# A fused attention and routed-expert kernel: group table ahead of places, group 1's weights asked for sooner, group 0's output in two halves, later sources marked beside group 1

## The reference

```python
attn_out = _attn_ref(...)                                  # B=4, H=8, S=576, D=64, causal softmax + linear memory
x = attn_out.transpose(0, 2, 1, 3).reshape(B * S, H * D)   # 2304 tokens x 512
# first mixture: each token goes to one expert of 8
logits = x @ w_gate + modality_bias[modality_id]
e_idx = argmax(logits); gate_w = softmax(logits)[e_idx]
for e in range(8):
    h = relu(x[e_idx == e] @ w1[e])                        # 512 -> 1024
    out[e_idx == e] = gate_w * (h @ w2[e])                 # 1024 -> 512
# second mixture: every expert on every token, weighted by P
P = exp(x @ w_gate2 - max);  8 times: normalise rows, then columns
out = sum_e P[:, e] * (relu(x @ w1b[e]) @ w2b[e])
```

## Time and profile before

| what | value |
|---|---|
| median of 3 timed runs | 2138.43 us (2133.97 to 2140.87) |
| the profiled execution, its own time | 2135.32 us |
| its span in the trace | 2133.7 us |
| PE busy / weight loads | 98% / 90% of the span |
| DVE, ACT, POOL busy | 69%, 42%, 36% |
| mean granted TensorE clock | 0.998 |

### The profile page before, as it was taken

The page is one execution under the profiler, slowest core; times in us unless marked ns, Lnnn a source line. Parts: engine busy times, 40 slices in busy tenths (PEclk is TensorE's granted clock), DMA queues, the critical chain, the costliest instruction groups (busy, mean ns, idle before and its releaser), DMA issues.

```text
span 2133.7 us, 35443 instructions
## 1 busy us (share of the span) xinstructions
PE 2092.5 (98%) x12113; PEld 1910.1 (90%) x12113; DVE 1469.6 (69%) x2929; ACT 902.2 (42%) x2050; POOL 762.3 (36%) x664
## 2 busy tenths in 40 slices
PE   8999998999999999999999999999999999999997
PEld 7999987999988998999889899989988998998996
DVE  7877777767776766666676666666667666666663
ACT  6766764554543433333343333334334333433341
POOL 4444443111332432343245234324425432442342
PEclk9999999999999999999999999999999999999999
DMA  5422224767632221122223122212222221222120
GB/s 119 144 53 66 68 80 160 247 227 222 212 100 83 66 80 60 60 80 75 63 61 109 60 60 80 77 58 64 79 65 85 80 76 58 65 80 64 56 79 30
DMA packets 158851, 194.65 MB, mean 91 GB/s; under 512 B 77025, under 2 KB 77025, under 8 KB 158689
## 3 DMA queue, kind: packets, MB, share of 16 engines
q1 hardware_dynamic: 151088, 171.27, 26.9%
q0 software_dynamic: 6400, 20.98, 2.8%
q10 hardware_dynamic: 1200, 0.30, 0.1%
HBM read 172.04 MB, written 20.45 MB: 90 GB/s over the span
## 4 chain that ended last, share of the span: by engine, by line
PE 79%; DVE 2%; issue 1%; DMA 1%; ACT 0%; POOL 0%; POOLq 0%; SPq 0%; ACTq 0%; DVEq 0%
PE b_pso L1746 12%; PE b_pso L1748 12%; PE b_pso L1747 12%; PE b_psp L1692 11%; PE b_psp L1695 11%; PE b_psp L1694 11%; PE b_pso L1135 2%; PE b_pso L1137 2%; PE b_pso L1136 2%; PE b_psp L1137 2%; PE b_psp L1136 2%; PE b_psp L1135 2%; PE b_psl L1670 1%; DVE b_hl L2253 1%; PE b_pst L1617 0%
## 5 line engine op out<-in xcount | busy, mean ns | idle before, releaser
L1532 POOL TENSOR_TENSOR b_w2l<-b_w2r,b_w2h 128x512 fp32r<-128x512 f32 x192 | 242.1, 1293 | 880.4 <-ACT b_w2h L1907 880.4
L1746 PE MATMUL b_pso<-b_w2h,b_hh 128*128 128x512 f32 x1152 | 449.8, 390 | 3.7 <-DVE b_acc L2323 3.3
L1692 PE MATMUL b_psp<-b_x,b_ah 128*128 128x384 f32 x1344 | 450.5, 335 | 1.7 <-ACT b_p1u L1943 1.7
L1695 PE MATMUL b_psp<-b_x,b_al 128*128 128x384 f32 x1344 | 449.8, 335 | 0.0
L1694 PE MATMUL b_psp<-b_x,b_ah 128*128 128x384 f32 x1344 | 449.6, 335 | 0.0
L1748 PE MATMUL b_pso<-b_w2h,b_hl 128*128 128x512 f32 x1152 | 449.4, 390 | 0.0
L1747 PE MATMUL b_pso<-b_w2l,b_hh 128*128 128x512 f32 x1152 | 449.1, 390 | 0.0
L2323 DVE SCALAR_TENSOR_TENSOR b_acc<-b_pso,b_prob,b_acc 128x512 f32<-128x512 f32 x252 | 189.1, 750 | 265.4 <-PE b_pso L1748 258.1
L1943 ACT ACTIVATE b_p1u<-b_psp 128x384 f32<-128x384 f32 x96 | 46.3, 483 | 580.8 <-PE b_psp L1695 580.8
L1746 PEld LDWEIGHTS b_pso<-b_w2h,b_hh 128*128 128x128 f32 x1152 | 216.3, 188 | 48.4 <-DVE b_acc L2323 4.2
L1692 PEld LDWEIGHTS b_psp<-b_x,b_ah 128*128 128x128 f32 x1344 | 252.3, 188 | 5.8 <-ACT b_p1u L1943 2.1
(11 more groups left out here) (351 smaller groups left out, 3844.8 us busy)
## 6 DMA issues: line engine op xcount, KB each, us to landing
dense_raw<-in_moe_w SPq DMA_DIRECT2D x192, 256.0 KB, 3.9
b_w2r<-in_moe_w SPq DMA_DIRECT2D x192, 256.0 KB, 2.9
weights_raw<-in_moe_w SPq DMA_DIRECT2D x176, 256.0 KB, 4.0
y_sorted<-r_y POOLq DMA_DIRECT2D x22, 256.0 KB, 4.0
y_sorted<-dense_raw SPq DMA_DIRECT2D x10, 512.0 KB, 4.0
weights_raw<-in_q SPq DMA_DIRECT2D x32, 128.0 KB, 2.4
weights_raw<-in_v SPq DMA_DIRECT2D x32, 128.0 KB, 2.5
x_tokens<-a_xs SPq DMA_DIRECT2D x4, 1024.0 KB, 4.5
```

Source lines behind the costliest of these rows:

```text
L1532: g_.tensor_tensor(w2l[:, j, :], w2r[:, j, :], w2h[:, j, :].bitcast(F32), ALU.subtract).then_inc(s_wl, 1)
L1692: t_.matmul(bank, ah[:, i, d, col], bh[i][:, d, :], start=(first and d == 0), stop=False, skip_group_check=True)
L1695: m = t_.matmul(bank, al[:, i, d, col], bh[i][:, d, :], start=False, stop=(d == CH - 1), skip_group_check=True)
L1746: t_.matmul(o, hh[:, f, tok], w2h[:, f, :], start=(q == 0), stop=False)
```

## The change

It has these parts. POOL makes the low parts of w1 chunks 0 to 3 of group 0 only; DVE makes 4 to 7, between `first_x_lo` and the last head's `weights`, and ACT's high parts of 4 to 7 move into the end of attention. `positions` is cut in two: `ends` (counts and ends of the groups) and the rest; `group_table` follows `ends`. `s_rwl` is now raised by POOL: 8 at once when both halves of w1 are split, then one for each w2 chunk, and SP asks for group 1's weights outside its loop. PE's output of group 0 goes in halves: tile 0 with f 0 to 3, the table for group 1's rows, tile 1 with f 0 to 3, tile 0 with f 4 to 7, both turns of group 1 (into banks of `b_psp`), tile 1 with f 4 to 7. Marking, table and `sources` for groups 2 and on move into group 1's hidden layer. POOL gathers group 2 outside its loop, after `sources`. Three register loads of PE move into the hidden layers of groups 2 to 4.

```diff
@@ attention, gpsimd_program
             for ch in range(4):
-                c["later"]["first_weights_lo"](pool, ch)
+                c["later"]["first_weights_lo_pool"](pool, ch)
             combine(NH - 2, B - 1, H - 2)
             combine(NH - 1, B - 1, H - 1)
-            for ch in range(4, 8):
-                c["later"]["first_weights_lo"](pool, ch)
@@ attention, scalar_program
             last_copied(2)
+            c["later"]["first_weights_hi"](act, 4)
             last_copied(3)
+            c["later"]["first_weights_hi"](act, 5)
...
@@ attention, vector_program
             for m in range(GT):
                 c["later"]["first_x_lo"](dve, m)
+                c["later"]["first_weights_lo"](dve, 4 + m)
             weights(NH - 1, NH // 2 - 1, H - 1)
+            c["later"]["first_weights_lo"](dve, 6)
+            c["later"]["first_weights_lo"](dve, 7)
@@ mixtures
-            return psp[:, 2 - m] if isinstance(g, int) and g == 0 else psx[:]
+            return psp[:, 2 - m] if isinstance(g, int) and g < 2 else psx[:]
...
-            if isinstance(g, int) and g == 0:
-                return (0, 1, 2, 3), (), (4, 5, 6, 7)
+            if isinstance(g, int) and g == 1:
+                return (0, 1, 2, 3, 4, 5), (), (6, 7)
@@ sync_program
+            sp.wait_ge(c["s_rt"], 1)
+            weights = c["expert_weights"](sp, route[0:1, 1:2])
+            for ch in range(NCH):
+                sp.wait_ge(s_rwl, ch + 1)
+                weights(ch)
             n = count(sp)
-            with sp.Fori(1, n) as g:
+            with sp.Fori(2, n) as g:
@@ gpsimd_program
+            def first_passed(f):
+
+                pool.wait_ge(s_rwl2, f + 1)
+                pool.sem_inc(s_rwl, 1)
+
+            pool.wait_ge(s_rwl0, DC)
+            pool.wait_ge(s_rwl1, DC)
+            pool.sem_inc(s_rwl, 2 * DC)
+            for f in range(FC):
+                first_passed(f)
             pool.wait_ge(c["s_xout"], 16 * 2 * B)
             pool.wait_ge(s_ix, 7)
             gather(1)
+            for f in range(FC, 2 * FC):
+                first_passed(f)
+            store(0)
             pool.wait_ge(s_idx, 3)
-            store(0)
+            gather(2)
+            pool.sem_inc(s_now, 1)
             n = count(pool)
             last, last2, last3 = count(pool, 1), count(pool, 2), count(pool, 3)
-            with pool.Fori(2, last2) as g:
+            store(1)
+            with pool.Fori(3, last2) as g:
@@ tensor_program
+            def first_output(m, half):
+
+                tok = slice(m * P, (m + 1) * P)
+                for f in range(half * FC, half * FC + FC):
+                    if m == 0:
+                        pe.wait_ge(s_rwl2, f + 1)
+                        pe.wait_ge(s_rhl, f + 1)
+                    i = split_matmuls(nc, pso[:, m, :], [
+                        (rhh[:, f, tok], rhl[:, f, tok], hi_of(2 * FC + f), lo_of(2 * FC + f))], f == 0, f == 2 * FC - 1)
+                if half:
+                    i.then_inc(s_ro, 1)
+            def beside_second(f):
+                if f == 5:
                     pe.wait_ge(s_part, 2)
                     table(psi, hotp, parts, LT * 2).then_inc(s_found, 1)
...
-            pe.wait_ge(r["s_red"], NH)
             pe.wait_ge(r["s_ptc"], 5 * NH)
             r_hidden(0, None, beside_hidden)
-            r_output(0, None, False, beside_output)
-            n = count(pe)
-            last, last2 = count(pe, 1), count(pe, 2)
-            r_hidden(1)
+            pe.wait_ge(r["s_red"], NH)
+            first_output(0, 0)
+            second_sources()
+            first_output(1, 0)
+            first_output(0, 1)
+            r_turn(1, 0)
+            r_turn(1, 1)
+            first_output(1, 1)
+            r_hidden(1, None, beside_second)
...
             for g in range(2, 5):
                 r_output(g - 1, g - 2, True, rows_table if g == 4 else None)
-                r_hidden(g)
+                r_hidden(g, None, a_count(("last", "last2", "n")[g - 2], (1, 2, 0)[g - 2]))
@@ vector_program
+            def y_copied(g, m):
+                dve.wait_ge(s_ro, RT * g + m + 1)
+                after(dve, s_st, 16 * RT * g)
+                v_.tensor_copy(y[:, m, :], pso[:, m, :]).then_inc(s_y, 1)
+
+            def beside_second(f):
+                rows_chain(f)
+                if f == 1:
+                    mark_tiles()
+                elif f == 2:
+                    mark_places()
+                elif f == 6:
+                    sources()
+
             w2_first(0)
+            w2_first(1)
             hidden_first(0)
-            w2_first(1)
             w2_first(2)
+            w2_first(3)
+            hidden_first(1)
             last_experts()
-            hidden_first(1)
-            w2_first(3)
             hidden_first(2)
+            ends()
+            group_table()
+            hidden_first(3)
             positions()
-            hidden_first(3)
             second_sources()
-            group_table()
-            for f in range(4, 8):
+            hidden_first(4)
+            gates()
+            second_rows()
+            w2_first(4)
+            for f in range(5, 8):
                 hidden_first(f)
                 w2_first(f)
-            dve.wait_ge(s_rwl0, 2 * FC)
-            dve.wait_ge(s_rwl2, 2 * FC)
-            dve.sem_inc(s_rwl, NCH)
-            mark_places()
-            gates()
-            sources()
-            r_ahead(1, 0, True)
-            r_first(1, rows_chain)
+            dve.wait_ge(s_rwl, NCH)
+            for ch in range(DC):
+                r_weights(1, ch)
+            y_copied(0, 0)
+            for m in range(RT):
+                r_x_lo(1, m)
+            for ch in range(DC, DC + 2):
+                r_weights(1, ch)
+            y_copied(0, 1)
+            for ch in range(DC + 2, 2 * FC):
+                r_weights(1, ch)
+            r_first(1, beside_second)
```

More of the change, by code:

```diff
@@ L853, in scalar_program @@
             last_copied(2)
+            c["later"]["first_weights_hi"](act, 4)
             last_copied(3)
+            c["later"]["first_weights_hi"](act, 5)
             c["later"]["first_x_hi"](act, 0)
+            c["later"]["first_weights_hi"](act, 6)
             c["later"]["first_x_hi"](act, 1)
@@ L858, in scalar_program @@
             copy_out(NH * NI - 1, H - 1, NH - 1)
+            c["later"]["first_weights_hi"](act, 7)
         def vector_program(dve):
@@ L1297, in mixtures @@
         s_rwl0 = sem("first_w1_lo")
+        s_rwl1 = sem("first_w1_lo_back")
         s_rwl2 = sem("first_w2_lo")
@@ L1614, in r_turn @@
                     pe.wait_ge(s_xg, 16 * RT * g)
-                pe.wait_ge(s_rxl, RT * g + m)
+                if isinstance(g, int) and g == 1:
+                    pe.wait_ge(s_rhl, 7 - m)
+                else:
+                    pe.wait_ge(s_rxl, RT * g + m)
                 for cc in range(DC):
@@ L1627, in r_hidden @@
                         if isinstance(g, int) and g == 0:
-                            pe.wait_ge(s_rwl0, DC * (f // FC + 1))
+                            pe.wait_ge(s_rwl1 if f else s_rwl0, DC)
                         else:
@@ L1651, in r_output @@
                         if m == 0:
-                            if isinstance(g, int) and g == 0:
-                                pe.wait_ge(s_rwl2, f + 1)
-                            else:
-                                pe.wait_ge(s_rwl, NCH * g + 2 * FC + f + 1)
+                            pe.wait_ge(s_rwl, NCH * g + 2 * FC + f + 1)
                             pe.wait_ge(s_rhl, 8 * g + f + 1)
@@ L1800, in beside_hidden, with a_count, also @@
                     last_ranks()
-                elif f == 7:
-                    second_sources()
-            def beside_output(m, f):
-                if m == 0 and f == 6:
+            def first_output(m, half):
[8 more added lines that the diff above has]
+                    i.then_inc(s_ro, 1)
+            numbers = {}
+            def beside_second(f):
+                if f == 5:
                     pe.wait_ge(s_part, 2)
                     table(psi, hotp, parts, LT * 2).then_inc(s_found, 1)
-                elif m == 1 and f == 1:
-                    r_turn(1, 0)
-                elif m == 1 and f == 5:
-                    r_turn(1, 1)
-            pe.wait_ge(r["s_red"], NH)
+            def a_count(name, less):
+                def also(f):
+                    if f == 3:
+                        numbers[name] = count(pe, less)
+                return also
             pe.wait_ge(r["s_ptc"], 5 * NH)
             r_hidden(0, None, beside_hidden)
-            r_output(0, None, False, beside_output)
-            n = count(pe)
-            last, last2 = count(pe, 1), count(pe, 2)
-            r_hidden(1)
+            pe.wait_ge(r["s_red"], NH)
[7 more added lines that the diff above has]
+            r_hidden(1, None, beside_second)
             def rows_table(m, f):
@@ L1830, in tensor_program @@
                 r_output(g - 1, g - 2, True, rows_table if g == 4 else None)
```

(17 more changed lines are left out.)

50 lines of the change are left out of this document (29 added, 21 removed).

## The result

| | kernel before | changed kernel |
|---|---|---|
| median of the runs | 2139.69 us (6 runs) | 2149.62 us (6 runs) |
| their range | 2133.97 to 2142.81 | 2148.47 to 2152.72 |
| mean granted clock of those runs | not on record (0.993 to 0.998 in the 50 executions beside the experiments) | 0.991 to 0.993 |
| profiled execution | 2135.32 us, clock 0.998 | 2150.77 us, clock 0.991 |

The ratio is 1.0051, with a 95% interval from 1.0036 to 1.0065: the change makes the kernel slower by some 10 us, twice what was forecast, and just past the end of the range. Of all the executions timed for this document one, of e8, ran at a mean clock of 0.654 and took 2969.54 us; it is in none of the ratios.

The account below looks back on a forecast made before the run. TensorE, busy 98% of the span, was taken as the bound, so only its gaps could be won. Terms: -5.9 us at T, +8.4 to U, +2.5 for the clock, 5.0 us slower: 2143.4 us, range 2135 to 2149.

Parts of the forecast that it names:

- T: First matmul of group 1's hidden layer; forecast at 360.3 against 366.22 before, a win of 5.9 us.
- U: Group 2's first turn; forecast at 381.2 against 378.70 before, 2.5 us late.
- group 2's rows become what is late: Sources made in group 1's hidden layer would delay group 2's gather; TensorE stands 8.7 us ahead of group 2's turn.
- the register loads in the later hidden layers: PE's three loads moved into hidden layers of later groups; taken at nothing, bound 1 us in all.
- the two landings: Gathers of groups 1 and 2, from second issue to rows landed; taken as about 4.3 and 4.5 us.
- from group 1's turns to T: Both turns of group 1 (0.75 us), then tile 1's second half of group 0's output (2.75 us).
- the clock behind U: After the 8.7 us wait TensorE would run 5 us at half pace, costing 2.5 us; bounds 0 to 4.2.
- the scale: Sum put on the profiled execution (2135.32 us), then 3.1 us added to reach the median of the runs.
- The second one: Rival: group 2's gather lands under full weight traffic, in 6.2 us; 1.7 us more, 2145.1; chance 0.12.
- The first: Rival: clock stays low as long as at the start, 8.3 us at half pace; 6.7 us slower, 2145.1; chance 0.17.
- The third: Rival: the clock does not fall, or comes back at once; 0 to 2.5 us slower, 2140.9 or less; chance 0.18.
- the fourth: Rival: group 2's rows come in time and the early gain is kept; 6.1 us less, 2132.3; chance 0.05.

Follow-up runs that it names:

- e8: Changed kernel with the edits of e1, e2 and e3, plus `sources` behind group 1's low parts of x: 2134.30 us, ratio 0.9981.
- e9: The kernel before, unchanged, profiled once more: 2139.72 us at a mean clock of 0.994.
- e10: The kernel before, unchanged, profiled another time: 2133.70 us at a mean clock of 0.998.
- e1: Changed kernel with later sources' marking ahead of group 1's first w1 low parts, their table ahead of its first turn, sources behind the first `r_y`: 2136.36 us, ratio 0.9991.
- e2: Changed kernel with POOL releasing group 1's w2 chunks only when group 1's rows have landed: 2147.16 us, ratio 1.0037.
- e3: Changed kernel with TensorE's wait for the last reduction put back ahead of group 0's hidden layer: 2147.76 us, ratio 1.0047.
- e5: Changed kernel with 56 turns of a 128x128 constant put into the wait ahead of group 2's first turn: 2152.13 us, ratio 1.0063.
- e6: Changed kernel with later groups' sources marked at f 0 and 1, TensorE's table at f 3, sources at f 4: 2145.78 us, ratio 1.0036.
- e4: Changed kernel with the edits of e1 and e2 together: 2136.91 us, ratio 0.9991.
- e7: Kernel before with only the wait for the last reduction moved behind group 0's hidden layer: 2139.88 us, ratio 1.0000.

## Why the prediction was wrong

The changed kernel's profile is set against e9, which has the same fall of the clock from 331 to 342. (e9 is not free of others: its clock is at 0.50 from 359 to 362.4, behind the 2.21 us wait for `r_parts`, and again from 666.2 to 669.6. Up to T they make little difference: e9 takes 27.9 us from the rank table, the profile before 27.4, e10 27.7.) Us between the marks:

| stretch | e9 | changed | difference | predicted |
|---|---|---|---|---|
| to the rank table | 341.19 | 340.77 | -0.4 | 0 |
| rank table to T | 27.9 | 26.1 | -1.8 | -5.9 |
| T to U | 12.35 | 22.30 | +9.95 | +8.4 |
| U to the last matmul's start | 1745.3 | 1748.4 | +3.1 | +2.5 |
| sum | | | +10.8 | +5.0 |

The medians differ by 9.9 us, so this account covers the result.

**Right: that group 2's rows become what is late, and by what chain.** The cast came 13.45 us behind T (predicted 14.3), the second issue 2.3 behind it (2.1), the wait was 10.0 us (8.7). e1 shows that with this chain undone the loss is gone. The chain from the rank table to group 1's cast took 11.5 us (11.6), group 1's w1 came in time, and the register loads in the later hidden layers leave no gap (TensorE busy 210.00 of 210 us from 395 to 605).

**Wrong, the step that failed: the two landings.** The prediction took 4.3 us for group 1's gather ("weights are now in flight too, so about 4.3") and 4.5 for group 2's. They took 7.1 (from 354.51 to 361.59) and 6.5: 2.8 and 2.0 us, 4.8 of the 5.8 by which the sum was short. The rows had the higher price: 6.2 us beside a DMA share of 1.04. It was kept for group 2 and a chance of 0.12. Group 1's landing was put between the quiet 3.9 and the loop's 4.6, though the same prediction brought its weights forward by some 11 us, and the weights' own traffic, from 344.94 to past the gather at 354.51, was never laid beside it. For group 1 e2 shows the cause and its size: with w2 held back the landing is at 3.9 us, and T comes 22.7 in place of 26.1 us behind the rank table. e8, with the same hold, has 3.9 to 4.3 us; e3 and e5, without it, have 6.1 to 7.1. On this the Trainium skill (DMA: Bandwidth & Descriptors, Queues, rings and completion order) says that each DMA engine takes turns between the queues that have work, packet by packet; e2's 3.9 against 6.7 us for group 1 agrees with it, though no row shows the turns themselves. For group 2 the size is measured and the cause is not shown: no run held the weights beside its gather, and e6 landed it in 4.1 us beside a DMA share of 0.89.

**Wrong: from group 1's turns to T.** The prediction gave this 3.5 us and counted the 1.56 us gap for group 1's last `r_xl` among those that go. It took 5.3 us (361.59 to 366.91), 1.8 more, and the clock was at 0.50 for 3.4 us of it, behind the 4.16 us wait: a second fall, where the prediction had one. But without that fall the stretch is hardly shorter. In e2 and e8, at a clock of 1.00, it took 5.1 us, 1.2 of them a wait for `r_xl`, and in e4 5.6 with 1.7. So at full clock TensorE stands for DVE instead, and the gap that was counted as won stays. These 1.8 us and the 4.8 of the landings are more than the 5.8 that were missing; the cast that came 0.85 us sooner behind T takes some of it back.

**About right: the clock behind U.** It cost 1.6 us up to group 2's second turn, inside the 0 to 4.2 on record and below its 2.5, and 2.7 us in e2. The rest of the 3.1 lies in the fall from 675 to 683, which other executions have as well, and shorter in e9: from U to the last matmul e7 took 1748.2 us, e9 1745.3 and e10 1743.5. The rule that the prediction cited (the Trainium skill, TensorE: Matmul & The Clock Gate, HAM oscillation — how this bites in real kernels), that a burst behind a wait for a transfer starts at half clock, held at U, where the clock was 0.50 all through the first turn, and from 0.2 us behind the end of the wait ahead of group 1; behind the 3.45 us left in e5 the first turn still ran at full pace. And the prediction's reading that waits of 2.2 us and less leave the clock at 1.00 was that of one execution: in e9 it fell 0.8 us behind the end of such a wait.

**Wrong: the scale.** The point was missed by 6.2 us, 4.9 of them in the change itself and 1.3 in the kernel before, whose median of six runs is 2139.69 where three had given 2138.43. The prediction put its sum on the profiled execution and added 3.1 us for the median, without asking what these were. They are, for the most part, falls of the clock inside work: e9, with those, took 6.0 us more than e10, without. Had it fallen only sometimes in the changed kernel too, the carry would have been fair; its six runs all lay at 0.991 to 0.993. Whether the change makes these falls more frequent, or six runs were too few to show an execution without them, stays open.

**The rivals.** The second one, group 2's gather landing in 6.2 us, is what happened (6.5), with its cause left open as said; it had not named group 1's gather, where the cause is shown. The first did not happen: the clock came back 3.3 us behind U, not 8.3. The third did not: the clock fell. Nor the fourth: group 2's rows came at T + 22.3, and nothing of T's gain was left.

## What to carry over

Before a transfer is asked for sooner, list what then shares the DMA with it, and price the next small gather at the busy landing, not at the quiet one; a load can be held by a wait on the gather's own semaphore, and in e2, e4 and e8 TensorE then waited for no weights. A chain that is moved off one gap must be followed to its own reader: work that had 21 us of slack became the longest wait of the kernel by being tied to T. And where the runs of a kernel differ by more than the change is worth, profile it twice, and compare executions with the same clock history.

## What was not expected of the hardware

TensorE's granted clock fell to 0.50 to 0.53 while TensorE was busy without a gap, beside 30 and 10 matmuls of 128x8 between products of 128x256 (331 to 342). It did so in e9 and not in e10, one program, and cost 3.0 us up to the rank table (4.1 less the 1.17 us by which e9 began later); e10 has a wait of 1.24 us for `hot` in that stretch and e9 none, so the matmuls themselves lost more. Of the 50 executions of the kernel before beside these experiments 17 had a mean clock of 0.997 or more and took 2133.4 to 2136.4 us; the other 33 took 2137.0 to 2143.3. Another fall stands where narrow logits lie between the first dense products: in the changed kernel (0.89 from 670 to 700), in e7 (0.90) and, a little sooner, in e9 (0.66 from 665 to 670), and not in e4, e8 or e10 (1.00). In the changed kernel and in e9 it began at the end of a wait of 1.3 us for DVE's `b_ring`; e4, e8 and e10 have that wait too, and no fall. What decides in which execution it comes was not found.
